# A two-MoE chain behind packed attention on one core: the first MoE's second product by blocks of 512 tokens instead of units of 288

## What is computed

```python
def sm_attn(qq, kk, vv):
    s = scale * np.matmul(qq, kk.transpose(0, 1, 3, 2))
    a = np.exp(s - np.max(s, axis=-1, keepdims=True))
    a = a / (np.sum(a, axis=-1, keepdims=True) + 1e-09)
    return np.matmul(a, vv)

p_packed = sm_attn(p, k, v)                  # 8 batches, 8 heads, 32 packed rows, head_dim 64
x = sm_attn(q, p_packed, p_packed)           # 576 queries per batch -> x: 4608 tokens x 512
h = x @ w_in1;  x = (h - np.tanh(h)) @ w_out1            # first MoE, d_ff 2048
h = x @ w_in2;  r = np.maximum(h, 0.0)
y = (s * (r * r) + b) @ w_out2                           # second MoE, d_ff 2048
```

## Time and profile before

| | |
|---|---|
| timed runs, median | 1457.78 us |
| profiled execution | 1456.46 us |
| its span | 1454.7 us |
| TensorE busy | 1446.1 us, 99% |
| VectorE busy | 871.4 us, 60% |
| ScalarE busy | 579.8 us, 40% |
| GpSimd busy | 80.3 us, 6% |
| DMA | 225.45 MB, mean 155 GB/s |

### The profile page before, as it was taken

One profiled execution on the slowest core, in us unless ns is written; L12 is line 12 of the kernel. 1 busy time (PEld: TensorE's weight loads), 2 busy tenths in 40 slices (PEclk: granted clock), 3 DMA queues, 4 the chain that ended last, 5 costly groups with the idle time before them and its releaser, 6 DMA issues.

```text
span 1454.7 us, 24312 instructions
## 1 busy us (share of the span) xinstructions
PE 1446.1 (99%) x9838; PEld 1270.3 (87%) x9838; DVE 871.4 (60%) x1582; ACT 579.8 (40%) x1116; POOL 80.3 (6%) x71
## 2 busy tenths in 40 slices
PE   8999999999999999999999999999999999999999
PEld 6989989899998989999998888888888888888887
DVE  6755555656566565558777545754557545754563
ACT  3444444444444444445544322632236322632243
POOL 3700100101010010000000000000000000000000
PEclk9999999999999999999999999999999999999999
DMA  9402321123222222032388554756467654756135
GB/s 350 166 9 83 115 82 63 55 83 113 82 82 86 72 75 72 18 104 75 125 319 294 219 210 159 275 207 252 170 224 253 223 204 159 275 209 257 62 126 192
DMA packets 79679, 225.45 MB, mean 155 GB/s; under 512 B 5584, under 2 KB 34384, under 8 KB 74960
## 3 DMA queue, kind: packets, MB, share of 16 engines
q1 hardware_dynamic: 79568, 223.89, 43.4%
HBM read 181.93 MB, written 41.94 MB: 154 GB/s over the span
## 4 chain that ended last, share of the span: by engine, by line
PE 99%; DMA 1%; SPq 0%; DVE 0%; issue 0%
PE banks L240 32%; PE banks L241 31%; PE banks L242 31%; PE banks L543 2%; DMA qT<-q_T 1%; PE banks L560 1%; PE banks L490 1%; PE banks L512 1%; PE banks L498 0%; PE banks L480 0%; PE banks L521 0%; PE banks L499 0%; SPq L282 0%; DVE y_store L1086 0%; SPq L289 0%; SPq L293 0%
## 5 line engine op out<-in xcount | busy, mean ns | idle before, releaser
L240 PE MATMUL banks<-g_high,w_out_parts 128*128 128x288 f32 x1024 | 310.2, 303 | 0.0
L242 PE MATMUL banks<-g_high,w_out_parts 128*128 128x288 f32 x1024 | 301.8, 295 | 0.0
L241 PE MATMUL banks<-g_low,w_out_parts 128*128 128x288 f32 x1024 | 301.5, 294 | 0.0
L879 ACT ACTIVATE g<-g,small 128x512 f32<-128x512 f32 x144 | 117.4, 815 | 294.5 <-DVE g L1254 293.8
L1168 DVE TENSOR_TENSOR g<-banks,g 128x288 f32<-128x288 f32 x256 | 116.8, 456 | 196.8 <-ACT g L828 195.3
L240 PEld LDWEIGHTS banks<-g_high,w_out_parts 128*128 128x128 f32 x1024 | 192.1, 188 | 39.0 <-issue 33.0
L240 PE MATMUL banks<-g_high,w_out_ring 128*128 128x512 f32 x576 | 224.4, 390 | 0.0
L241 PE MATMUL banks<-g_low,w_out_ring 128*128 128x512 f32 x576 | 224.3, 389 | 0.0
L242 PE MATMUL banks<-g_high,w_out_ring 128*128 128x512 f32 x576 | 224.2, 389 | 0.0
L828 ACT ACTIVATE g<-banks 128x288 f32<-128x288 f32 x256 | 105.2, 411 | 274.7 <-PE banks L242 272.4
L242 PEld LDWEIGHTS banks<-g_high,w_out_parts 128*128 128x128 f32 x1024 | 192.3, 188 | 0.0
(11 more groups left out here) (155 smaller groups left out, 1974.9 us busy)
## 6 DMA issues: line engine op xcount, KB each, us to landing
w_out_ring<-w_out_parts_scratch SPq DMA_DIRECT2D x144, 512.0 KB, 4.2
w_in_first<-w_in_operands_scratch SPq DMA_DIRECT2D x28, 1792.0 KB, 7.4
kT<-k_T SPq DMA_DIRECT2D x16, 576.0 KB, 4.0
qT<-q_T SPq DMA_DIRECT2D x16, 576.0 KB, 6.2
x1T_scratch<-x_store SPq DMA_DIRECT2D x16, 576.0 KB, 3.8
v_rows<-v_rows SPq DMA_DIRECT2D x8, 1024.0 KB, 5.8
w_out_parts_scratch<-w_out_stage SPq DMA_DIRECT2D x16, 512.0 KB, 2.7
out_T<-y_store SPq DMA_DIRECT2D x8, 1024.0 KB, 6.8
```

The lines of the kernel that those rows point to most:

```text
L240: nc.tensor.matmul(out, high, rhigh, start=first, stop=False)
L241: nc.tensor.matmul(out, high, rlow, start=False, stop=False)
L242: return nc.tensor.matmul(out, low, rhigh, start=False, stop=last)
L879: nc.scalar.activation(TG2[:, cc % 2, :], TG2[:, cc % 2, :], ACT.Identity, bias=b_col, scale=s_col).then_inc(g_done, 1)
```

## The change

The second product of the first MoE no longer follows the units of 288 tokens. g of a whole batch (16 chunks x 576 tokens) is kept in SBUF (`g1`, `G`); the first 512 tokens of each batch form a block, and the last 64 tokens of the eight batches (`LEFT`) are written to HBM (`store_left`) and come back at the end as a ninth block (`load_left`). `second(gc)` is numbered over both MoEs, 9 x 16 chunks each, and issues 12 matmuls of 512 columns. It starts at step 18 and stands at every even step (`second_at`); the parts of chunk i of batch b are made at step 32b + 16 + 29i/15 (`PARTS_AT`: `high_g1`, `low_g1`). In steps 0 to 15 `first1` uses four banks and runs up to four steps ahead of g.

Room for g comes from two streams. w_out1's parts now pass through the ring of four slots: in the first block GpSimd splits each row block in its slot, SyncE stores the parts to HBM, and the blocks after it load them from there (512 KB each). w_in1 has two slots of one quarter each (1024 KB, plus two more at the start) and is loaded again for every batch. SyncE's queue is written by even steps; `load_w_in1(6)`, the third quarter for batch 1, stands at step 26. The tables of steps for attention are new (`AT_FIRST`, `AT_NEXT`), and `O` is copied at step 16 (`COPY_AT`). The conversion of w_in2 for the second MoE is partly moved into the 25 second products that remain after step 255. The output's columns are put back in order on the host.

```diff
+def second_at(c):
+    return c // 2 - FC // 2 - 1 if c >= FC + 2 and c % 2 == 0 else None
...
+PARTS_AT = {2 * FC * b + FC + (29 * i) // 15: FC * b + i for b in range(B) for i in range(FC)}
+SECOND_TAIL = second_at(STEPS1 - 2) + 1
+PARTS_TAIL = max(s for c, s in PARTS_AT.items() if c < STEPS1) + 1
...
+MIX_AT = {12: 0, 15: 1, 18: 2, 21: 3}
...
+AT_FIRST = dict(s1=(9, 11), max1=(12, 12), exp1=(13, 14), t1=(14, 16), stats1=17, packed=18, packed_t=20, s2=22,
+                max2=23, sub2=24, exp2=25, sum2=26, norm2=27, back2=28, high2=29, low2=30, m=(24, 26, 28))
...
+COPY_AT = FC
...
+    W1 = at("w_in1_ring", [P, 2, KX, BANK], F32, WIN_AT + 30208)
...
+    WR = at("w_out_ring", [P, RING, 2, DM], F32R, WR_AT)
+    WR_RAW = at("w_out1_raw", [P, RING, 2, DM], F32, WR_AT)
+
+    G = at("g1", [P, FC, S], F32, G_AT)
...
-            def load_w_in1(n):
-                sp.dma_start(W1[:, :, n * BANK:(n + 1) * BANK],
-                             w_in1[n:KX * NB:NB, :, :].rearrange("k p f -> p k f")).then_inc(w_in1_in[n], 16)
+
+            def load_w_in1(k):
+                n, first = k % NB, k in (2, 3)
+                if k >= NB:
+                    sp.wait_ge(m_done, k - 3 if k < 6 else k - 1)
+                sp.dma_start(w1_rows(k), w_in1[n:KX * NB:NB, :, :].rearrange("k p f -> p k f")
+                             ).then_inc(w_in1_first[k - 2] if first else w_in1_in[k % 2], 16)
...
+            def next_w_out(gc):
+                if gc < FC:
+                    store_w_out1(gc)
+                take = gc + RING
+                if take < NS1 + NU2 * FC:
+                    second_done(sp, gc)
+                    if gc < FC:
+                        sp.wait_ge(w_out1_out, 16 * (gc + 1))
+                    if take < FC:
+                        load_w_out1(take)
+                    else:
+                        rows = w1_dram if take < NS1 else w2_dram
+                        sp.dma_start(read(WR[:, take % RING, :, :]),
+                                     rows[take % FC, :, :].rearrange("p (a f) -> p a f", a=2)
+                                     ).then_inc(w_ring_in[take % RING], 16)
+
+
+            def store_left(b):
+                sp.wait_ge(g_done, 2 * FC * (b + 1))
+                sp.dma_start(left_dram[:, :, b * LEFT:(b + 1) * LEFT], G[:, :, U2:S]).then_inc(left_out, 16)
+
+            def load_left(k):
+                sp.wait_ge(left_out, 16 * B)
+                sp.wait_ge(low_done, NS1 - 2 * FC + 4 * k + 4)
+                sp.dma_start(G[:, 4 * k:4 * k + 4, 0:U2], left_dram[:, 4 * k:4 * k + 4, :]).then_inc(left_in[k], 16)
...
+                if second_at(c) is not None:
+                    next_w_out(second_at(c))
                 if b >= 1:
-                    store_x(2 * b - 1)
+                    if m == 2:
+                        store_left(b - 1)
+                    if m == 20:
...
+                    if m in ((6, 10, 26, 28) if b == 0 else (2, 22, 26)):
+                        load_w_in1(4 * b + ({6: 4, 10: 5, 26: 6, 28: 7} if b == 0 else {2: 5, 22: 6, 26: 7})[m])
+                    if m == 30 and b + 2 < B:
+                        load_w_in1(4 * b + 8)
...
-            def second1(c):
-
-                unit, i = divmod(c, FC)
-                pe.wait_ge(low_done, c + 1)
-                pe.wait_ge(w_out1_ready, i + 1)
-                if c == 0:
+            def second(gc):
+
+                blk, i = divmod(gc, FC)
+                pe.wait_ge(low_done, gc + 1)
+                if gc < FC:
+                    pe.wait_ge(w_out1_ready, i + 1)
+                else:
+                    pe.wait_ge(w_ring_in[gc % RING], 16 * (gc // RING - FC // RING + 1))
+                if gc == 0:
                     pe.wait_ge(mb_ready, 2)
+                    pe.wait_ge(g_done, FC)
                 for d in range(KX):
                     if i == 0:
-                        wait(pe, (o_copied_act, o_copied_dve)[d % 2], 2 * unit - 1 + d // 2)
+                        wait(pe, (o_copied_act, o_copied_dve)[d % 2], 2 * blk - 1 + d // 2)
                     cols = slice(d * P, (d + 1) * P)
-                    last = product(O[:, d, 0:U1], WOUT[:, i, 0, cols], WOUT[:, i, 1, cols],
-                                   GH1[:, c % RING, :], GL1[:, c % RING, :], i == 0, i == FC - 1)
+                    last = product(O[:, d, :], WR[:, gc % RING, 0, cols], WR[:, gc % RING, 1, cols],
+                                   GH[:, gc % RING, :], GL[:, gc % RING, :], i == 0, i == FC - 1)
                     if i == FC - 1:
...
-            for c in range(STEPS1 + LAG):
-                if c < STEPS1:
-                    first1(c)
-                    side(c)
-                if c >= LAG:
-                    second1(c - LAG)
+            for c in range(STEPS1):
+                first1(c)
+                side(c)
+                if second_at(c) is not None:
+                    second(second_at(c))
+            for gc in range(SECOND_TAIL, NS1 - 1):
+                second(gc)
             seven(0, 0)
+            second(NS1 - 1)
...
+            def high_g1(s):
+                blk, i = divmod(s, FC)
+                if s == 0:
+                    act.wait_ge(m_done, NB)
+                if blk < B:
+                    act.wait_ge(g_done, 2 * FC * blk + FC + i + 1)
+                else:
+                    act.wait_ge(left_in[i // 4], 16)
+                if s >= RING:
+                    second_done(act, s - RING)
+                nc.scalar.copy(GH[:, s % RING, :], G[:, i, 0:U2]).then_inc(high_done, 1)
...
+            def low_g1(s):
+                dve.wait_ge(high_done, s + 1)
+                nc.vector.tensor_tensor(GL[:, s % RING, :], G[:, s % FC, 0:U2], read(GH[:, s % RING, :]), ALU.subtract
+                                        ).then_inc(low_done, 1)
...
-                nc.vector.tensor_tensor(TG1[:, c % 2, :], HB[:, c % 2, 0:U1], TG1[:, c % 2, :], ALU.subtract
-                                        ).then_inc(g_done, 1)
+                if b >= 1 and u == 0:
+                    dve.wait_ge(low_done, FC * (b - 1) + i + 1)
+                if b >= 1 and u == 1:
+                    dve.wait_ge(left_out, 16 * b)
+                nc.vector.tensor_tensor(G[:, i, u * U1:(u + 1) * U1], banks[:, hb(c), 0:U1], TG1[:, c % 2, :],
+                                        ALU.subtract).then_inc(g_done, 1)
...
-                dve.wait_ge(high_done, c + 1)
-                nc.vector.tensor_tensor(GL1[:, c % RING, :], TG1[:, c % 2, :], read(GH1[:, c % RING, :]),
-                                        ALU.subtract).then_inc(low_done, 1)
-
-                if i == 1 and w >= 1:
-                    copy_o(w - 1, 3, OS1, U1, x1_out, 16 * (w - 1))
+                if c in PARTS_AT:
+                    low_g1(PARTS_AT[c])
+
+                if b >= 1 and m == COPY_AT:
+                    copy_o(b - 1, 1)
+                    copy_o(b - 1, 3)
```

571 lines of the change are left out of this document (279 added, 292 removed).

## The result

The changed kernel takes 1483.88 us (median of four runs, 1481.99 to 1487.65), the kernel before 1457.44 us in the same comparison: a ratio of 1.0183, 95% interval [1.0161, 1.0206]. It is slower by 26 us where I forecast 5.8 us faster, and 24 us above the upper end of the range. The profiled execution took 1481.99 us, its span 1480.2 us.

A forecast was written before the change was run, and what follows sets the result against it. TensorE's own instructions were taken to bound the kernel: 1456.5 - 16.0 + 3.5 + 5.1 + 1.5 = 1450.6 us, 1451.9 on the timed runs' scale, so 1452. The 8 in 10 range was 1441.5 to 1460.

The forecast's parts named there:

- what I cost at nothing: Low part's chain, ring refills, GpSimd's splits, ninth block and handover to the second MoE: all taken as covered, 0 us.
- part three: w_in1 reloaded per batch: TensorE waits 4.7 and 0.4 us for M blocks 2 and 3 of batch 1, +5.1 us.
- Rival 3: Ring starves: late landings in SyncE's one queue delay second products; 1466 us at landings of 13.3 us; chance 0.09.
- Part one: First MoE's second product in blocks of 512: 1344 fewer instructions for the same columns, -16.0 us.
- Part two: First 18 steps: TensorE waits on attention and VectorE work before the first 512-wide matmul at 49 us, +3.5 us.
- Part four: Handover between blocks, step 16 of batches 1 to 6: scores of step 18 wait 0.25 us six times, +1.5 us.
- The last batch: End of the first MoE: ninth block's products and work moved into the 25 last second products, taken to cost nothing.
- Rival 2: Clock falls at the long w_in1 wait, to half rate for about one pair of steps: 1455.5 us; chance 0.15.
- The forecast's own mechanism: Fewer, wider matmuls on TensorE less three small sets of waits: 1452 us, own range 1448 to 1455, chance 0.43.

The follow-up runs named there:

- both edits: Changed kernel with stores of w_out1's parts two parts ahead and w_in1's two loads ahead of the ring refill: 1459.22 us, 1.0017 of the kernel before.

## Why the prediction was wrong

**The step that failed** is in "what I cost at nothing": "The first 16 parts are split by GpSimd in 2.5 us each while a ring slot has three pairs of steps." It counts the split and leaves out what SyncE does with each part: store, wait for the landing, refill. Those stood in the diff. I priced the refills (4.2 us against 12.9) as if they were issued when the slot was free; in the first block each is issued only after its slot's store has landed (median 6.2 us from issue to landing, up to 9.4 in the chain), and the next store only after that. Three pairs of steps are the cover of one slot and are used up once. One in-order queue serves all slots, so what had to be set against one pair of steps, 5.0 us, was the queue's time for one part: 7.3 us. As an estimate from these rows: over 15 parts the queue falls behind by 33 us, the cover takes 12.9 of it, and some 20 are left; TensorE idled 20.3 us.

The price: 128.4 us for the stretch against 101.6 with the stores moved by one part and w_in1's loads ahead, **26.8 us**, about 20 of them idle TensorE (20.3 against 0.1 from 50 to 200 us) and the rest slower matmuls (clock 0.94 against 1.00). In the medians both edits gave back 24.7 us: 16.6 by the stores alone, 20.5 by the stores once w_in1's loads stood ahead. Of the whole only the 5.1 us of part three had been priced.

**Rival 3** named the queue ("one late wait in that queue delays all behind it") but asked for late landings by traffic, 13 us and more, and put the price over the whole first phase. The ring's loads from HBM landed in a median of 4.1 us, as before (4.2); what was late was the issue of refills, in the first 16 of 144 chunks. It got 0.09.

**Part one**, -16.0 us: the price of a start is right to 0.1 ns. Per batch it should give 7.4 us; 6.75 are there.

**Part two**, first 512-wide matmul at 49 us: it starts at 48.79 in the profiled run. The 1.5 us waited at the transposes of step 14 is 1.96. Such a close match is in part luck: in the profiles of three later versions with the same tables for the start it comes at 48.92, 50.76 and 53.20.

**Part three**, 4.7 + 0.4 us near 73 us: mis-sized in the kernel as changed, 7.45 + 0.58 at 81.7 us, since the load's issue was late by the chain. With the stores two ahead and this order kept it is 5.80 + 1.52 = 7.3 us against 5.1: the load took 6.5 us to land, not 5.8, and the clock fell. The mechanism, a load queued behind its step's refill, is shown by the reversal: with the loads ahead 0.7 us of waiting were left, and the median fell by 8.1 us. "In later batches the loads are six steps ahead (10.9 us) or more, and hidden" failed once, for M block 2 of batch 2: its load went out at 165.21, as planned, and landed 13.96 us later, since SyncE had just caught up and put eight other transfers, some 4.7 MB, ahead of it in 4.4 us. With the stores ahead this wait is gone.

**Part four**, 1.5 us: the gap before the scores of step 18 is 0.43 us where the M blocks of the same batch have 0.21, after:

```profile
236.82 0.29 PE L271 MATMUL banks<-probs2T_parts,m_parts 128*128 128x288 f32 x1
237.25 0.72 PE L648 MATMUL banks<-qT,packedT 64*32 64x288 f32 x16
```

so 0.2 us for each batch, as sized. The other 0.4 to 0.5 us by which a batch misses the 7.4 I did not forecast and did not take apart.

**The last batch** I cost at nothing. From its M block 3 on, the matmuls that are left come to 878.7 us (an estimate: 31 first products of 6 and 41 second products of 12 at the prediction's prices, 2.0 us for the block and the scores, and the 740.5 us that the second MoE took before); the kernel took 885.6. Of the 6.9 us between, 3.04 are the wait for the ring; spreading what stood ahead of it took 4.3 us off the median, 2.3 of them shown in the profile.

**Rival 2**, the clock: it does fall at such waits (0.73 behind 7.45 us, and no dip where nothing waited, 200 to 600 us). The Trainium skill (TensorE: Matmul & The Clock Gate, section Loop structure matters more than you think) says so, and the trace agrees. Its price at the M block is 1.1 to 1.6 us, not the 3 to 4 I gave it, and keeping the clock up gave nothing in the end.

**The forecast's own mechanism** is nearly what remains when the queue is mended: 1453.8 us against 1452 forecast. That is luck: part three is not in that version, and without its 5.1 us the forecast would be 1446.9. The missing tenths per batch (some 2 to 3 us) and the rest of the tail (3 to 4 us) stand in its place.

## What to carry to other kernels

Where a ring gets a store as well as a load in one in-order queue, write down for one item what the queue does, and add the landings that are waited for. Set that sum against the time in which the kernel uses up one item (here 7.3 us against 5.0), not against the cover of a slot, which is used up once. Then look what stands ahead of each store: other loads of the same step lengthen the landing that is waited for (6.9 to 9.4 us in place of 3.9 to 5.0). Placing the next store straight behind the refill, an edit of a few lines, was enough here. The total that a queue waits says little: 89 us hurt and 59 us didn't; look whether TensorE's list names anything that stands behind it.

The wait itself had to stay in all these versions, since the refill overwrites what the store reads. The Trainium skill (DMA: Bandwidth & Descriptors, section Two DMAs through the same engine are not ordered) speaks of a transfer that reads what an earlier one writes; for a dependent transfer it advises to wait on the first one's semaphore before the second is issued. Here the dependence is the other way round, a refill over what a store still reads, and the kernel waits in the same way. No run here tried it without.
